# Passage from the attention and feed-forward units to the expert slots: reordered work of unit 35, and a later start of the raw expert pieces

## The reference, cut to what matters

```python
x = attention(q, k, v)                       # 4608 tokens x 512
h = x @ w_in                                 # 4608 x 1024
solu = h * softmax(h)
ln = (solu - mean(solu)) / sqrt(var(solu) + 1e-6) * g_ln
x = ln @ w_out                               # 4608 x 512
logits = x @ w_gate; e_idx = argmax(logits)
gate_w = softmax(logits)[e_idx]; eom = 1 / (1 + exp(-(x @ w_output_gate)))
for e in range(8):
    rows = e_idx == e
    out[rows] = gate_w * eom[rows, e] * (relu(x[rows] @ w1[e]) @ w2[e])
```

## Time and profile before

| | |
|---|---|
| median of 3 runs | 1044.69 us (1044.49 to 1044.91) |
| the profiled execution | 1042.38 us |
| its span, first to last instruction | 1040.6 us |
| PE busy | 1012.6 us, 97% of the span |
| DVE, ACT, POOL busy | 545.7, 403.1, 256.9 us |
| mean granted clock of PE | 0.997 of full speed |

### The profile page before, as it was taken

How to read it: one execution, slowest core, us unless ns; L and a number is a source line. 1 busy time by engine, 2 the same in 40 slices (tenths; PEclk the granted TensorE clock), 3 DMA queues, 4 the chain that set the end, 5 groups by cost and what they waited for, 6 DMA issues and landing times.

```text
span 1040.6 us, 24250 instructions
## 1 busy us (share of the span) xinstructions
PE 1012.6 (97%) x7323; PEld 839.2 (81%) x7324; DVE 545.7 (52%) x1137; ACT 403.1 (39%) x733; POOL 256.9 (25%) x458
## 2 busy tenths in 40 slices
PE   5899999999999999999999999999999999999997
PEld 4788888888888888888877888888888888888885
DVE  5677767677676777676636533234333332342521
ACT  5544434444444444344432434234242432342521
POOL 5772202113121312021222222212212121122211
PEclk9999999999999999999999999999999999999999
DMA  8442322323222322222014444233232331341110
GB/s 294 157 163 82 50 86 70 82 82 82 61 66 79 82 82 61 73 73 62 22 51 159 147 149 144 90 93 122 90 121 91 112 122 51 100 127 55 32 42 30
DMA packets 43024, 97.15 MB, mean 93 GB/s; under 512 B 9678, under 2 KB 9806, under 8 KB 42960
## 3 DMA queue, kind: packets, MB, share of 16 engines
q1 hardware_dynamic: 31616, 75.51, 23.4%
q0 software_dynamic: 9248, 20.70, 6.2%
q10 hardware_dynamic: 2096, 0.04, 0.1%
HBM read 76.66 MB, written 20.60 MB: 93 GB/s over the span
## 4 chain that ended last, share of the span: by engine, by line
PE 94%; DMA 2%; issue 2%; DVE 1%; ACT 1%; POOL 0%; SPq 0%; POOLq 0%; ACTq 0%; DVEq 0%
PE Y_ps L442 39%; PE H_ps L442 39%; PE X L434 8%; PE S L434 3%; PE S L530 2%; PE X L544 2%; PE L_ps L518 1%; DMA stage<-in_moe_w_in 1%; DMA xg<-x_rows,slot_rec 1%; POOL route_table L1271 0%; ACT stage L712 0%; DVE nmax_h L900 0%; DVE dl L877 0%; DMA route_table<-rec,posi 0%; SPq L331 0%
## 5 line engine op out<-in xcount | busy, mean ns | idle before, releaser
L442 PE MATMUL Y_ps<-wx,dh 128*128 128x512 f32 (+1 forms) x1200 | 382.3, 400 | 0.5 <-DVE dl L877 0.5
L442 PE MATMUL H_ps<-wx,xh 128*128 128x512 f32 (+1 forms) x1216 | 334.6, 397 | 2.9 <-DVE xl L877 2.3
L442 PEld LDWEIGHTS H_ps<-wx,xh 128*128 128x128 f32 x1216 | 223.5, 189 | 46.1 <-issue 2.4
L442 PEld LDWEIGHTS Y_ps<-wx,dh 128*128 128x128 f32 x1200 | 217.6, 189 | 43.3 <-DVE dl L877 0.8
L442 PE MATMUL Y_ps<-wx,dl 128*128 128x512 f32 (+1 forms) x600 | 235.2, 392 | 0.0
L442 PE MATMUL H_ps<-wx,xl 128*128 128x512 f32 (+1 forms) x608 | 187.9, 390 | 0.0
L877 DVE TENSOR_TENSOR dl<-X,dh 128x512 fp32r<-128x512 f32 x152 | 97.6, 683 | 81.1 <-ACT dh L689 80.8
L877 DVE TENSOR_TENSOR wx<-stage,wx (+1 forms) x58 | 70.4, 1224 | 122.9 <-ACT wx L843 120.3
L442 PEld LDWEIGHTS H_ps<-wx,xl 128*128 128x128 f32 x608 | 114.4, 188 | 24.5
L442 PEld LDWEIGHTS Y_ps<-wx,dl 128*128 128x128 f32 x600 | 112.9, 188 | 24.8
L900 DVE TENSOR_REDUCE nmax_h<-H_ps 128x1 f32<-128x1024 f32 x36 | 44.0, 1224 | 85.6 <-PE H_ps L442 85.6
(11 more groups left out here) (194 smaller groups left out, 1011.1 us busy)
## 6 DMA issues: line engine op xcount, KB each, us to landing
stage<-in_experts SPq DMA_DIRECT2D x64, 512.0 KB, 3.5
stage<-in_q SPq DMA_DIRECT2D x36, 256.0 KB, 3.0
stage<-in_k SPq DMA_DIRECT2D x36, 256.0 KB, 3.7
stage<-in_v SPq DMA_DIRECT2D x36, 256.0 KB, 3.6
x_rows<-x SPq DMA_DIRECT2D x36, 256.0 KB, 2.0
stage<-in_moe_w_out SPq DMA_DIRECT2D x4, 512.0 KB, 5.6
stage<-in_moe_w_in SPq DMA_DIRECT2D x3, 512.0 KB, 7.1
slot_rec<-route_table POOLq DMA_DIRECT2D x40, 2.0 KB, 2.7
```

Of the source, the lines that this page charges most:

```text
L442: i = pe.matmul(acc[:, c0:c0 + HALF], x[:, kk, :], w(part, kk * cols + c0), start=first and x is hi and part == 0, stop=last and x is lo)
```

## The change

In the kernel after, unit 35's transposes leave the common step for PE's tail, and there the lower half (X_ps) goes first, ahead of the upper half (T1). ACT makes the dh copies of unit 35 (lower first) before it copies x2 of unit 34, and DVE takes the lower half first. The transposes of slot 0's gathered rows go ahead of unit 35's second layer. That layer sums in L_ps instead of Y_ps; its first four blocks need only the lower half, and the transposes of unit 34's x2 stand in its middle. DVE splits slot 0's rows ahead of copying unit 34's x2T. In slot 2 (`first_late`: s + 1 == EARLY) the transposes of slot 3's gathered rows move from ahead of the second layer of slot 1 to its middle. SP's first six raw pieces wait for slot 3's gather to have landed, instead of for the routing records.

```diff
@@ sync
-            sp.wait_ge(rec_st, 16 * NT)
+            sp.wait_ge(xg_in[EARLY % 2], 32)
             for i in range(RING - 2):
                 load_raw(RING + i, first_raw[i])
@@ tensor, step
-                if has(0) and not (isinstance(s, int) and s == 0):
+                if has(0) and not (isinstance(s, int) and s in (0, NT - 1)):
                     hidden_rows(s)
@@ tensor, tail
-                pe.wait_ge(x2_ev, NT - 1)
-                pe.wait_ge(dl0_ev, NT); pe.wait_ge(dl1_ev, NT)
+                pe.wait_ge(cen_done, NT)
+                pe.wait_ge(xl_ev, NT)
+                transposed(X_ps, [cen[:, i * P:(i + 1) * P] for i in range(4)], ident[:, :]).then_inc(th0_tp, 1)
                 pe.wait_ge(x2T_ev, NT - 2)
-                outputs(NT - 2, 0)
+                transposed(T1, [cen[:, HALF + i * P:HALF + (i + 1) * P] for i in range(4)], ident[:, :]).then_inc(th1_tp, 1)
+                pe.wait_ge(xg_in[0], 16)
+                pe.wait_ge(ssub, NT)
+                gathered(xg[0])
+                pe.wait_ge(dl0_ev, NT)
+                pe.wait_ge(rt_rec, NCH - 1)
                 for kk in range(KF):
-                    if kk == 5:
-                        pe.wait_ge(xg_in[0], 16)
-                        pe.wait_ge(ssub, NT)
-                        gathered(xg[0])
-                    i = products(Y_ps, (dh, dl), DM, lambda part, c0: wts(1, part, 1, c0, HALF), kk, kk == 0, kk == KF - 1)
+                    if kk == KF // 2:
+                        pe.wait_ge(dl1_ev, NT)
+                        pe.wait_ge(x2_ev, NT - 1)
+                        outputs(NT - 2, 0)
+                    i = products(L_ps, (dh, dl), DM, lambda part, c0: wts(1, part, 1, c0, HALF), kk, kk == 0, kk == KF - 1)
                 i.then_inc(mm2_done, 1)
...
                 first_layer(1)
+                pe.wait_ge(x2_ev, NT)
                 logits(NCH)
@@ tensor, slot
-                if has(1):
+                first_late = isinstance(s, int) and s + 1 == EARLY
+
+                def next_rows():
+
                     pe.wait_ge(xg_in[(u + 1) % 2], uses(c, u + 1, 2) * 16)
                     gathered(xg[(u + 1) % 2])
+                if has(1) and not first_late:
+                    next_rows()
...
                                 hidden_half(s, 0)
+                            if first_late:
+                                next_rows()
                             pe.wait_ge(g1_lo, s)
@@ scalar, step
-                if has(-1):
+                if has(-1) and not (isinstance(s, int) and s == NT - 1):
@@ scalar, tail
-                dh_parts(NT)
+                act.wait_ge(mm2_done, NT - 1)
+                act.wait_ge(th0_tp, NT)
+                copy(dh[:, 0:4, :], quad(X_ps), dh0_ev)
+                act.wait_ge(th1_tp, NT)
+                copy(dh[:, 4:8, :], quad(T1), dh1_ev)
+                act.wait_ge(xs_done, NT - 1)
+                act.wait_ge(st_x2[0], (NT // 2 - 1) * 16)
+                act.wait_ge(x2_tp, NT - 3)
+                act.activation(x2[0][:, :], Y_ps[:, :], ACT.Copy, scale=xscale[:, 0:1]).then_inc(x2_ev, 1)
                 act.wait_ge(mm1_done, NT)
                 rows(0)
...
-                act.activation(x2[1][:, :], Y_ps[:, :], ACT.Copy, scale=xscale[:, 0:1]).then_inc(x2_ev, 1)
+                act.activation(x2[1][:, :], L_ps[:, :], ACT.Copy, scale=xscale[:, 0:1]).then_inc(x2_ev, 1)
@@ vector, tail
             dve.wait_ge(mm2_done, NT - 1)
+            dve.wait_ge(dh0_ev, NT)
+            less(dl[:, 0:4, :], quad(X_ps), dh[:, 0:4, :], dl0_ev)
             dve.wait_ge(dh1_ev, NT)
             less(dl[:, 4:8, :], quad(T1), dh[:, 4:8, :], dl1_ev)
-            dve.wait_ge(dh0_ev, NT)
-            less(dl[:, 0:4, :], quad(X_ps), dh[:, 0:4, :], dl0_ev)
-            outputs(NT - 2)
             dve.wait_ge(mm1_done, NT)
             rows(0)
+            outputs(NT - 2)
             outputs(NT - 1)
```

## The result

The kernel after takes 1038.62 us (median of 6 runs, 1038.06 to 1038.92), before 1044.67 us in the runs beside it: ratio 0.9938, 95% interval 0.9927 to 0.9949.

The account below looks back on a forecast made before the run. PE bounds the kernel (94% of the span), so only its waits and lower clock count. Gains of 1.4 and 3.85 us less a 1.65 us stall make 3.6 us: 1044.69 to 1041.1 us, range 1039.0 to 1043.4.

Parts of the forecast that it names:

- The first gap was followed by no lower clock: PE's 2.0 us wait at unit 35, before unit 34's x2 transposes: no lower clock after it, so none was priced.
- on the median 1044.69 - 3.6: Whole kernel: the summed gain of 3.6 us taken off before's median, giving 1041.1 us.
- my sum had 1.7 us for it: Gap before slot 3's rows: lower clock costs 4.0 - 2.33 = 1.7 us beyond the wait.
- Part 1: Unit 35 in PE's tail: lower half first lets the second layer start near 529.3; gain 1.4 us.
- Part 2: Slot 3's rows: gather lands about 3.2 us after its start, removing PE's wait and lower clock; gain 3.85 us.
- 0.15 us for slot 1's dl: Slot 1's second layer: waiting for dl's lower half takes 0.15 off the 4.0 us excess at slot 3's rows.
- The rival by which the gather was slow by itself: Slot 3's gather still takes 6.2 us, pieces go later, 3.3 us more stall: gain 0.3, 1044.4; chance 0.05.
- Part 3: Cost of late pieces and late rows: PE stalls 1.65 us at slot 2's dl, near 575.3 to 577.0.
- What I had called harmless: Raw pieces 14 and later: 14 follows at 574 to 576, 15 4.3 us later; later pieces have slots to spare.
- the stall: PE's wait at slot 2's dl: 1.65 us, bounds 0 and 2.7 us.
- part 1 at nothing: Rival at unit 35: copies start no earlier, ACT held by squares until 527.7; gain 2.2, 1042.5; chance 0.08.
- a fall added by the change: Rival at slot 2's dl: the stall drops the clock, costing 1.7 us; gain 1.9, 1042.8; chance 0.13.

Follow-up runs that it names:

- both gaps filled: Kernel before plus 18 idle transposes in PE's gap at unit 35 and 18 before slot 3's rows, no wait changed: 1041.68 us against 1044.47 (0.9974).

## Why the prediction was wrong

**The step that failed** is that on the clock, in two sentences: "The first gap was followed by no lower clock", and the sum "on the median 1044.69 - 3.6". I took one execution, 2.3 us below its median, as the rule, and carried its saving over to the others. In the ordinary execution the fall also comes at unit 35, where it costs 1.6 us (8.01 against 6.40 us to slot 0's first layer). The saving there is waits plus clock. Filling both gaps takes away 2.8 us, which is the lower clock; my sum had 1.7 us for it, at one of two places, and nothing at the other. From both gaps filled to after 3.0 us more are saved (1041.68 to 1038.68, on one chip), where my sum had 1.9 us for the waits and what is given back.

That last 1.1 us stays open. The first two profiles bear the sum out: 3.4 us less one fall of 1.5 us leaves 1.9. The profile with both gaps filled is at least no clean picture of before without falls, since slot 3's rows come to PE 8.65 us after slot 2's first layer there, and 8.06 us after it in the first profile.

**Part 1.** 1.4 us forecast, 1.15 to 1.2 in the profile: the second layer began at 529.35 (529.3 forecast) and slot 0's first layer at 535.45 (535.2). Right to 0.25 us, but for the clock: alone it brought 1.9 us by the medians.

**Part 2.** The gather took about 3.3 us (start 557.85, piece 8 at 562.22 one microsecond after it), 3.2 forecast; slot 3's first layer came at 570.00, 569.4 forecast. That the 3.2 us came so near is in part luck: the rows had the bytes of slot 2's gather and of the store beside it moved 3.75 us after the start (535.55 to 539.3), and none gave 3.2. The 3.85 us came out as 3.5. The sum took off 0.15 us for slot 1's dl, but the rows now stand inside the second layer, which takes 6.84 us with them (563.16 to 570.00) and 6.37 without (580.60 to 586.97). The rival by which the gather was slow by itself fell: apart from raw pieces it takes 3.4 us, among them 6.2 in before, with nothing else changed but SP's wait. By the rule of turns in the Trainium skill, "DMA: Bandwidth & Descriptors", Queues, rings and completion order, raw pieces would hardly slow the gather; here they did, from 3.4 to 6.2 us. Whether POOL's queue always had work in that time, which the rule supposes, no run shows.

**Part 3.** 1.65 us forecast at slot 2's dl; PE was held there for 0.4 us (6.34 us from slot 3's first layer to the second layer of slot 2, 5.92 before), 0.23 us of it by slot 4's rows. Of the difference of 1.2 us, 0.6 us is only that PE itself came later than forecast (570.00, not 569.4). The rest was in the sum, where the way from the first splits to the second is too long: scaling came 0.1 us before the splits ended and the second splits at 571.67, not 572.3, and DVE did four splits without a gap in 4.75 us from 570.94. What I had called harmless cost 0.8 us instead in this profile: piece 14 was issued at 577.1, not at 574 to 576, since six pieces landed later than by the old pace, and piece 15 came too late. That the sum of 3.6 met 3.4 is luck: 1.2 us too much for the stall stood against 0.25 us too much for part 1, 0.35 for part 2 and 0.8 us that was left out.

**The range** held part 1 at nothing and a fall added by the change, but no case in which the kernel before loses more to the clock than its profile shows. The evidence for that case stood in the first table: 1042.38 and 1044.69.

## What to carry to other kernels

Before a saving read from a profile is subtracted from a median, ask why the two differ; where they do, the profile is one draw of several, and a gap of PE near the length after which its clock fell elsewhere must be priced with and without the fall. To find out, fill the gap with idle transposes: if useless work makes the kernel faster, the rest of the gap's price was the clock. A transfer on which PE waits was worth keeping free of bulk loads here, even though the wait of the issuing queue delayed those by 6 us; then follow the last of the delayed loads, not only the first.

## What the runs showed of the hardware

The same gap of 2.0 us was followed by the lower level of PE's clock (0.81 and 0.90 over 12 us) in one execution of the same program and not in another, and a gap of 0.7 us by none in the six profiles that have it. Of the six profiles with the gap of 2.0 us unfilled, four had the fall after it and two had not; of the four with 2.2 to 2.9 us before slot 3's rows, three had it and one had not. One fall cost 1.5 to 1.6 us.

The Trainium skill, "TensorE: Matmul & The Clock Gate", Part 1, says that the number of slow matmuls at the start of one kernel varies from run to run. The traces agree in kind, and show it after gaps in the middle of a kernel: the executions of before, ordered by their mean clock, go from 1041.1 us (0.999) to 1047.0 us (0.992). After, without the two gaps, varied between 1038.0 and 1040.2 us.

Slot 3's gather of 256 KB landed 3.3 to 3.4 us after its start with no bulk load in flight, and 5.9 to 6.7 us after it among loads of 512 KB from another queue.
